# Moving VectorE's x_low, transpose and w_s4 steps within the second stage's model products (attention, then two MLPs)

## The reference

```python
scores = cap * np.tanh(scale * (q @ k.T) / cap)           # 2 x 12 heads, 448 x 64
attn = softmax(scores); x = attn @ v                      # then x: 896 tokens x 768
h = x @ w_in;  g = np.maximum(h, 0) ** 2;  x = g @ w_out  # first MLP, 768 -> 2048 -> 768
h = x @ w_in2; g = h / (1 + np.exp(-h));   out = g @ w_out2   # second MLP
```

## Time and profile before

| | |
|---|---|
| median of 3 runs | 532.03 us |
| the profiled execution | 531.69 us |
| its span | 529.9 us |
| PE busy | 521.0 us (98%) |
| DVE busy | 350.9 us (66%) |
| ACT busy | 260.3 us (49%) |
| granted clock of TensorE, mean | 0.999 of 2.4 GHz |

### The profile page before, as it was taken

The page is one execution under the profiler, slowest core; times in us unless marked ns, Lnnn a source line. Parts: engine busy times, 40 slices in busy tenths (PEclk is TensorE's granted clock), DMA queues, the critical chain, the costliest instruction groups (busy, mean ns, idle before and its releaser), DMA issues.

```text
span 529.9 us, 7052 instructions
## 1 busy us (share of the span) xinstructions
PE 521.0 (98%) x2628; PEld 440.0 (83%) x2628; DVE 350.9 (66%) x604; ACT 260.3 (49%) x404; POOL 77.5 (15%) x52
## 2 busy tenths in 40 slices
PE   7999999999999999999999999999999999999996
PEld 5333335799999999999999999999999999999996
DVE  3487878797687533667799746556764245568975
ACT  5999996154454333544444344454444144454220
POOL 1899999000000000000000000000000000000000
PEclk9999999999999999999999999999999999999999
DMA  7798611051302202522032025202211241020447
GB/s 222 196 241 227 180 41 33 28 141 59 80 0 80 59 1 59 141 59 67 13 80 61 1 61 139 61 18 62 60 49 32 61 138 36 26 80 10 102 74 106
DMA packets 82181, 42.17 MB, mean 80 GB/s; under 512 B 26848, under 2 KB 79072, under 8 KB 82144
## 3 DMA queue, kind: packets, MB, share of 16 engines
q1 hardware_dynamic: 77984, 40.32, 29.2%
q10 hardware_dynamic: 4128, 1.38, 1.1%
q0 software_dynamic: 32, 0.00, 0.0%
HBM read 38.93 MB, written 2.75 MB: 79 GB/s over the span
## 4 chain that ended last, share of the span: by engine, by line
PE 94%; DMA 2%; DVE 1%; ACT 1%; issue 1%; SPq 1%; ACTq 0%
PE banks L558 27%; PE banks L557 27%; PE banks L559 27%; PE banks L477 4%; PE banks L470 4%; PE banks L498 2%; PE banks L467 1%; DMA qk_raw<-in_k_dram 1%; DMA qk_raw<-in_q_dram 1%; PE banks L489 1%; ACT prob L683 1%; SPq L324 1%; ACT prob L690 0%; DVE asum L917 0%; ACTq L660 0%
## 5 line engine op out<-in xcount | busy, mean ns | idle before, releaser
L557 PE MATMUL banks<-x_hi,w_hl 128*128 128x448 f32 x384 | 139.4, 363 | 0.0
L558 PE MATMUL banks<-x_lo,w_hl 128*128 128x448 f32 x384 | 139.4, 363 | 0.0
L559 PE MATMUL banks<-x_hi,w_hl 128*128 128x448 f32 x384 | 138.3, 360 | 0.0
L558 PE MATMUL banks<-g_lo,w_hl 128*128 128x448 f32 (+1 forms) x340 | 122.7, 361 | 0.0
L557 PE MATMUL banks<-g_hi,w_hl 128*128 128x448 f32 (+1 forms) x340 | 122.5, 360 | 0.0
L559 PE MATMUL banks<-g_hi,w_hl 128*128 128x448 f32 (+1 forms) x340 | 121.7, 358 | 0.0
L557 PEld LDWEIGHTS banks<-x_hi,w_hl 128*128 128x128 f32 x384 | 72.1, 188 | 6.9 <-issue 1.4
L559 PEld LDWEIGHTS banks<-x_hi,w_hl 128*128 128x128 f32 x384 | 71.8, 187 | 5.1
L558 PEld LDWEIGHTS banks<-x_lo,w_hl 128*128 128x128 f32 x384 | 72.1, 188 | 3.8
L975 DVE TENSOR_TENSOR w_hl<-w_raw,w_hl 128x768 fp32r<-128x768 f32 x32 | 31.9, 996 | 55.4 <-ACT w_hl L716 55.2
L557 PEld LDWEIGHTS banks<-g_hi,w_hl 128*128 128x128 f32 x340 | 63.8, 188 | 4.8
(11 more groups left out here) (63 smaller groups left out, 509.8 us busy)
## 6 DMA issues: line engine op xcount, KB each, us to landing
w_raw<-in_moe_w_in_dram SPq DMA_DIRECT2D x32, 384.0 KB, 3.4
w_raw<-in_moe_w_out_dram SPq DMA_DIRECT2D x24, 512.0 KB, 5.2
qk_raw<-in_k_dram SPq DMA_DIRECT2D x44, 112.0 KB, 2.7
qk_raw<-in_q_dram SPq DMA_DIRECT2D x44, 112.0 KB, 3.3
v_t<-in_v_dram SPq DMA_DIRECT2D x24, 96.0 KB, 2.8
out_dram<-rows SPq DMA_DIRECT2D x38, 56.0 KB, 2.2
qk_raw<-in_k_dram ACTq DMA_DIRECT2D x4, 112.0 KB, 3.0
qk_raw<-in_q_dram ACTq DMA_DIRECT2D x4, 112.0 KB, 4.0
```

What stands on the lines that cost most here:

```text
L557: pe.matmul(dst, hi[:, kk, :], mov_hi, start=start, stop=False, skip_group_check=onto)
L558: pe.matmul(dst, hi[:, kk, :], mov_lo, start=False, stop=False, skip_group_check=onto)
L559: return pe.matmul(dst, lo[:, kk, :], mov_hi, start=False, stop=stop, skip_group_check=onto)
```

## The change

Only the order of VectorE's queue in stage 1 of each layer's model products changes; no instruction is added or removed. `leave` does nothing in stage 0, so stage 0 has the same order as before.

```diff
                     w_s2(layer, s, 1)
                     prod_low(layer, s, 1, 1)
+                    leave(layer, s, 0, 0)
+                    leave(layer, s, 0, 1)
                     take(layer, s, 0, 5)
                     if s == 1:
                         prod_low(layer, s, 1, 2)
...
                         end = last and layer == 1 and s == 1
+                        if s == 1:
+                            take(layer, s, g - 1, 6)
                         if s == 0 or g > 1:
                             prod_low(layer, s, g, 2)
+                        w_s4(layer, s, g)
+                        leave(layer, s, g - 1, 2)
                         if s == 1:
-                            take(layer, s, g - 1, 6)
                             take(layer, s, g, 0)
-                        w_s4(layer, s, g)
                         prod_low(layer, s, g, 3)
-                        if g == 1:
-                            leave(layer, s, 0, 0)
-                            leave(layer, s, 0, 1)
+                        leave(layer, s, g - 1, 3)
                         if s == 1:
                             take(layer, s, g, 1)
                         prod_low(layer, s, g, 4)
-                        leave(layer, s, g - 1, 2)
                         if s == 1:
                             take(layer, s, g, 2)
                         prod_low(layer, s, g, 5)
-                        leave(layer, s, g - 1, 3)
```

## The result

The changed kernel takes 535.63 us (median of 4 runs, 535.09 to 537.03) against 532.07 before: a ratio of 1.0061, 95% interval 1.0049 to 1.0075. Run again beside the kernel before it took 535.09 against 532.17, ratio 1.0050, interval 1.0037 to 1.0063. The forecast was 535.1. Its profiled execution took 535.17 us with a span of 533.4, against 529.9. Medians here and in the table leave out slow executions, of which there was one, of the one-leave kernel: 881.09 us at a granted clock of 0.558.

What follows compares the result with a forecast made beforehand. TensorE, busy without a gap in both second stages, was taken to bound the kernel. Two stalls of about 1.5 us, taken as 3.1 together, on the median 532.03 gave 535.1 us, slower by 0.6%; range 534.2 to 536.3.

Steps and rivals of the forecast that it cites:

- TensorE has no idle time to win: Second stages of both layers: TensorE busy 42.00 of 42.00 us, so no reordering of VectorE can make it faster.
- The deadline and its slack of 0.65 us: Group 1, both layers: take(1,0) ends 0.65 us ahead of the first weight load of product (1,2), which needs it.
- Added time of 2.20 and 2.24 us: Three leaves and w_s4 ahead of take(1,0) add 2.20 us in layer 0, 2.24 in layer 1; take about 1.55 late.
- From lateness to stall: Ahead of product (1,2): 1.55 + 0.05 - 0.08 gives a TensorE stall of 1.5 us per layer, two taken as 3.1.
- the release: Time from the end of VectorE's step to TensorE's waiting load, taken as 0.05 us from the end of the attention.
- the 0.08 of the restart: After idling, TensorE's second matmul starts 0.31 us after the first load, against 0.39 in steady flow: 0.08 given back.
- The weight load is not pulled ahead of the wait: First load of (1,2): a load behind a semaphore wait does not run early, as seen at 95.74.
- other sum: If the first load of (1,2) ran before the wait ended, each stall would be 0.19 us shorter, the sum 2.7.
- Group 2, prod_low and the stores cost nothing: No stall at (2,2), 0.65 us in hand in layer 0; prod_low in time; tail of about 4 us, at most 0.3 less.
- The clock stays up: During the stalls TensorE's granted clock stays at 1.00, as about 3 us of idleness passed before it fell at the end.
- That rival: The clock falls in the gap, so one product per stall takes 4.8 instead of 2.4 us: 539.9 us, chance 0.03.
- Rival 3: The debt also reaches product (2,2): a lag of 1.2 us adds 0.6 in each layer, 536.3 us, chance 0.07.

Runs made afterwards that it cites:

- one-leave kernel: Kernel before, with w_s4 and then leave(0,0) moved ahead of take(1,0) in group 1 of stage 1: 533.32 us, ratio 1.0015.
- group-2 kernel: Kernel before, with only group 2 in the new order: 532.00 us, ratio 0.9991.
- take-first kernel: Changed kernel, with group 0's leaves put behind take(1,0) and take(2,0) put ahead of w_s4: 532.04 us, ratio 0.9992.
- w_s4 alone: Kernel before, with w_s4 and take(1,0) exchanged in group 1 of stage 1: 532.23 us, ratio 1.0002.
- long gap: Kernel before, with eight chained scratch-tile additions put ahead of take(1,0) in both layers: 544.86 us, ratio 1.0233.

## Why the prediction was right

- *TensorE has no idle time to win:* it held. No kernel of the study was below 518.96 from start to last transpose.
- *The deadline and its slack of 0.65 us in both layers:* it held. Over five kernels with a stall and the clock up, it is the time put ahead less 0.61 to 0.69, where the terms give 0.61 (the larger values are layer 1's, where the take behind a transpose is 0.03 shorter, as read): in layer 0 2.21 gave 1.59, 1.13 gave 0.52, 1.07 gave 0.46, 0.61 gave nothing, 3.18 gave 2.55.
- *Added time of 2.20 and 2.24 us, take(1,0) 1.55 late:* it held, at 2.21 and 2.25. Layer 0 has the take's end at 282.14 against a load that would have been at 280.58, 1.56 late. Each of the three leaves found its input ready, as VectorE's row has no gap ahead of any.
- *From lateness to stall:* the release was mis-sized, 0.12 us (282.14 to 282.26) where I took 0.05 from the end of the attention; the 0.08 of the restart came back as read (282.57 - 282.26 = 0.31). Two stalls were 3.15 instead of 3.1. Why this release is longer than that one, no run shows.
- *The weight load is not pulled ahead of the wait:* it held. The prediction's other sum, 2.7 us, had the load done early. The Trainium skill ("TensorE: Matmul & The Clock Gate", section "Architectural detail") only says that loads are pulled ahead of matmuls in flight; whether one passes a wait, it leaves open. The trace has the load 0.12 us after the take's end in both layers, and not beneath the last matmul before the stall: it did not pass the wait.
- *Group 2, prod_low and the stores cost nothing:* it held, shown by the group-2 kernel and, for prod_low(1,3), by the take-first kernel. The 0.65 us in hand for take(2,0) measured 0.66. The tail from the last transpose's end to the end of the span went from 3.45 to 3.36 us, with spans given to 0.1 us; that is inside the 0.3 allowed.
- *The clock stays up:* it held for gaps of this length, and still for 2.6 us. That rival's mechanism is real, though: at a stall of 4.6 us it added 4.1 us over the two layers. The Trainium skill's "TensorE: Matmul & The Clock Gate" (section "Part 1: The HAM clock gate") says that the clock follows how busy TensorE has recently been; the trace agrees, with 1.00 throughout at 2.6 and 0.50 at 4.6.
- *Against the median:* the forecast set 3.1 on 532.03. The first set of runs gave 3.6, the second 2.9; the stalls were 3.15 and 3.16 in the two profiled executions (1.59 and 1.56, then 1.59 and 1.57), so the difference is the spread of the medians. All 15 executions listed with the first result have a median of 535.16. That the repeat came out at 535.09 beside a forecast of 535.1 is closer than the spread allows, and so partly luck.
- *Slips in the working that changed nothing:* the upper bound of a stall by its own terms is 1.55 + 0.05 + 4 x 0.1 = 2.0 us and not 1.9, and of both 4.0, which makes 536.0, still inside the range. The old order had 1.26 us in hand at take(2,0) of layer 0 (its pair ended at 295.70), which is 0.6 more than the new one, not 1.2 more. Rival 3 charged 0.6 us in each layer, though the prediction's own numbers leave take(2,0) of layer 1 some 1.26 us, so a lag of 1.2 would have cost only layer 0.

## What to carry to other kernels

Where one engine is busy without a gap, give each step of the others a deadline, the start of the instruction that waits for it, and compare the ends with it; a mean load of 80% on the other engine says nothing about a slack of 0.65 us. A step that frees a bank belongs ahead of the steps that nobody waits for: the same leaves and w_s4 cost 3.15 us ahead of the take and nothing behind it. A stall is the lateness plus the release less what the restart gives back; this line held to 2.6 us, and at 4.6 the clock had fallen and the price was higher.

## What the runs showed that I had not expected

A wait for VectorE's PSUM read released TensorE's weight load 0.11 to 0.12 us after the take's end (six kernels with a stall and the one with w_s4 alone), where the one for an SBUF addition at the end of the attention took 0.05. Eight chained additions ran at a pitch of 5.16 / 8 = 0.645 us, 0.11 more than the 0.53 from one take to a next step that needn't wait for it. And the clock can fall after the work has begun again: in layer 1 of the long gap at 509, three matmuls into the product.
